# Fusion kernel on one core: Gate's weights multiplied into the second layer's weights, and the logits taken as 8 more columns of the second layer from the second block on

## What is computed

```python
h = x @ w_in
g = np.where(h > 0.0, h, alpha * (np.exp(np.minimum(h, 0.0)) - 1.0))
x2 = g @ w_out                       # 1536 x 384
logits = x2 @ w_gate                 # 1536 x 8
expert_idx = np.argmax(logits, axis=1)
probs = np.exp(logits - logits.max(-1, keepdims=True))
probs /= probs.sum(-1, keepdims=True) + 1e-09
gate_w = probs[np.arange(N), expert_idx]
# a token's row goes to the next free slot of its expert (capacity 384); then per expert
# out = gate_w * (max(row @ w1, 0) @ w2)
```

## Time and profile before

| | us |
|---|---|
| runs of the kernel before (3) | 440.31, 440.59, 441.05; median 440.59 |
| the profiled execution: time | 441.02 |
| the profiled execution: span of the trace | 439.3 |
| PE busy in it | 418.8 (95%) |
| VectorE, ScalarE, GpSimd busy | 244.7, 183.2, 232.5 |
| mean granted clock of PE | 0.999 |

### The profile page before, as it was taken

The page is one execution under the profiler, slowest core; times in us unless marked ns, Lnnn a source line. Parts: engine busy times, 40 slices in busy tenths (PEclk is TensorE's granted clock), DMA queues, the critical chain, the costliest instruction groups (busy, mean ns, idle before and its releaser), DMA issues.

```text
span 439.3 us, 9249 instructions
## 1 busy us (share of the span) xinstructions
PE 418.8 (95%) x3604; PEld 399.6 (91%) x3604; DVE 244.7 (56%) x595; ACT 183.2 (42%) x390; POOL 232.5 (53%) x240
## 2 busy tenths in 40 slices
PE   7779999999999999999999999988999999999994
PEld 7669989999999999899999999866999999999994
DVE  7867864665466536744664477573455365463521
ACT  4356643333332333233333445334455564564520
POOL 1888776549554965396533334114343825627431
PEclk9999999999999999999999999999999999999999
DMA  6993978204210411030008000721826638458100
GB/s 242 399 411 87 367 247 297 76 17 131 64 49 17 133 52 60 1 101 2 1 15 327 1 1 37 286 91 31 313 95 265 244 127 328 152 196 313 44 30 26
DMA packets 16825, 62.36 MB, mean 142 GB/s; under 512 B 2044, under 2 KB 9510, under 8 KB 14737
## 3 DMA queue, kind: packets, MB, share of 16 engines
q1 hardware_dynamic: 14992, 57.08, 36.1%
q0 software_dynamic: 1792, 4.73, 2.9%
HBM read 49.38 MB, written 13.21 MB: 142 GB/s over the span
## 4 chain that ended last, share of the span: by engine, by line
PE 65%; DVE 11%; POOL 9%; issue 8%; ACT 3%; DMA 3%; SPq 0%; POOLq 0%; DVEq 0%; ACTq 0%
PE bank L1193 18%; PE bank L1195 18%; PE bank L1194 17%; POOL g_lo L596 3%; ACT elu L726 2%; DVE elu L1027 2%; PE bank L1355 2%; DVE wd_lo L922 2%; DMA rkt<-rkt 1%; POOL slots L574 1%; DVE wd_lo L928 1%; DMA nat<-nat 1%; DVE elu L1030 1%; PE bank L1342 1%; POOL rku L518 1%
## 5 line engine op out<-in xcount | busy, mean ns | idle before, releaser
L596 POOL TENSOR_TENSOR g_lo<-elu,g_hi 128x256 fp32r<-128x256 f32 x95 | 75.1, 790 | 99.5 <-ACT g_hi L728 98.3
L726 ACT ACTIVATE elu<-elu 128x256 f32<-128x256 f32 x96 | 40.2, 419 | 109.3 <-DVE elu L1027 109.0
L1193 PE MATMUL bank<-xt,wd_hi 128*128 128x256 f32 x288 | 81.7, 284 | 4.0 <-DVE elu L1030 2.0
L1195 PE MATMUL bank<-xt,wd_lo 128*128 128x256 f32 x288 | 81.0, 281 | 0.0
L1194 PE MATMUL bank<-xt,wd_hi 128*128 128x256 f32 x288 | 81.0, 281 | 0.0
L1193 PE MATMUL bank<-wd_hi,g_hi 128*128 128x384 f32 x192 | 67.4, 351 | 0.0
L1030 DVE SCALAR_TENSOR_TENSOR elu<-elu,bank 128x256 f32<-128x256 f32 x96 | 40.4, 421 | 47.9 <-ACT elu L726 47.9
L1027 DVE TENSOR_SCALAR elu<-bank 128x256 f32<-128x256 f32 x96 | 40.3, 420 | 47.0 <-PE bank L1195 46.6
L1194 PE MATMUL bank<-wd_lo,g_hi 128*128 128x384 f32 x192 | 64.5, 336 | 0.0
L1195 PE MATMUL bank<-wd_hi,g_lo 128*128 128x384 f32 x192 | 64.4, 336 | 0.0
L1193 PEld LDWEIGHTS bank<-xt,wd_hi 128*128 128x128 f32 x288 | 54.1, 188 | 6.2 <-DVE elu L1030 3.3
(11 more groups left out here) (199 smaller groups left out, 956.6 us busy)
## 6 DMA issues: line engine op xcount, KB each, us to landing
we_raw<-wexp SPq DMA_DIRECT2D x8, 1536.0 KB, 7.1
wd_raw<-wexp SPq DMA_DIRECT2D x8, 1536.0 KB, 7.5
nat<-nat SPq DMA_DIRECT2D x10, 672.0 KB, 4.9
rkt<-rkt SPq DMA_DIRECT2D x12, 512.0 KB, 6.8
xrow<-slots SPq DMA_DIRECT2D x16, 193.0 KB, 7.3
wd_raw<-win SPq DMA_DIRECT2D x4, 768.0 KB, 8.6
wd_raw<-wout SPq DMA_DIRECT2D x4, 768.0 KB, 10.6
slots<-blank SPq DMA_DIRECT2D x1, 2702.0 KB, 12.6
```

The lines of the kernel that those rows point to most:

```text
L596: nc.gpsimd.tensor_tensor(g_lo[:, f % 4, :], elu[:, f % 2, :], g_hi[:, f % 4, :].bitcast(F32), ALU.subtract).then_inc(s_glo, 1)
L726: nc.scalar.activation(elu[:, f % 2, :], elu[:, f % 2, :], ACT.Exp).then_inc(s_exp, 1)
L1193: mm(dst, w_hi, x_hi, start=start, stop=False)
L1195: return mm(dst, w_lo, x_hi, start=False, stop=stop)
```

## The change

Gate's weights are multiplied into w_out on the chip, once, in block 0: for this SP loads the transposed w_out (3.1 MB, `wo_tr`), and PE runs 12 plain f32 products of 32 by 512 (`gated_w_out`, tile 11), ScalarE copies the result, PE transposes it in four pieces (`gated_transpose`, tile 13), and ScalarE and VectorE split it into 8 columns that stand ahead of the 384 of each tile of w_out in `wd_hi` and `wd_lo` (128 x 16 x 8 numbers). The rows of w_out in these tables are thus 392 long (`WO`), and the four loads of w_out land in pieces of 384 numbers. Gate's weights are padded to 32 columns. From block 1 on `fc2` has 392 columns, and the logits are the first 8 columns of the copied rows (`x2row`, now 394 long). Only the logits of block 0, in block 1, are still made by transposes and products of their own. For the later blocks the transposes, their copies and the logits' products are gone, and the routing steps move: `shift` to tile 3, `choose` 5, `gates` 6, `count` 7, `place_rows` 8, the scatters 9 and 10. After block 5 the same steps are gone, the others keep their order. The diff, cut to its core:

```diff
+    WO = NE + DM
+    GP = 32
+    NG = 128 // GP
+    GCOL = DFF // NG
...
-    gate_w = new("gate_w", [128, KT, NE])
+    gate_w = new("gate_w", [128, KT, GP])
-    x2row = [new(f"x2row{b}", [128, BT, XR]) for b in range(2)]
+    x2row = [new(f"x2row{b}", [128, BT, NE + XR]) for b in range(2)]
...
-    wd_hi = new("wd_hi", [128, 2 * WI], F32R)
+    wd_hi = new("wd_hi", [128, WI + FT * WO], F32R)
...
-        F_T, F_LG, F_CHOOSE, F_GATE, F_CNT, F_SLOT, F_SCAT = 3, 6, 7, 8, 8, 9, 10
+        F_T, F_LG = 3, 6
+        F_WG, F_WGT = 11, 13
+        def route(n):
+            return dict(zip(("shift", "choose", "gates", "count", "place", "scatter"),
+                            (6, 7, 8, 8, 9, 10) if n == 0 else (3, 5, 6, 7, 8, 9)))
...
             def load_out(i):
                 cols = slice(i * WCOL, (i + 1) * WCOL)
-                sp.dma_start(wd_raw[:, WI + i * WCOL:WI + (i + 1) * WCOL], wout[:, cols]).then_inc(s_wld2[i], 16)
+                at = WI + i * WCH * WO
+                sp.dma_start(wd_raw[:, at:at + WCH * WO].rearrange("p (f c) -> p f c", f=WCH)[:, :, NE:WO],
+                             wout[:, cols].rearrange("p (f c) -> p f c", f=WCH)).then_inc(s_wld2[i], 16)
...
             for c in range(4, NSTEP):
                 load_rkt(c)
+                if c == 4:
+                    sp.dma_start(wo_tr[:, :, :], wouttr).then_inc(s_wtl, 16)
                 load_nat(c)
...
+            def gated_copy():
+                act.wait_ge(s_wg, 1)
+                nc.scalar.copy(wg_tr[:, :], ps_s[0][:, :]).then_inc(s_wgt, 1)
+            def gated_hi():
+                act.wait_ge(s_wgb, 1)
+                nc.scalar.copy(gate_part(wd_hi), gate_bank()).then_inc(s_wghi, 1)
...
+            def gated_lo():
+                dve.wait_ge(s_wghi, 1)
+                V.tensor_tensor(gate_part(wd_lo), gate_bank(), gate_part(wd_hi).bitcast(F32),
+                                ALU.subtract).then_inc(s_wglo, 1)
...
-                dve.wait_ge(s_lg, n + 1)
-                L = ps_lg.rearrange("p (t e) -> p t e", t=BT)
+                if n == 0:
+                    dve.wait_ge(s_lg, 1)
+                    L = ps_lg.rearrange("p (t e) -> p t e", t=BT)
+                else:
+                    for t in range(BT):
+                        dve.wait_ge(s_x2[t], n + 1)
+                    L = x2row[n % 2][:, :, 0:NE]
...
-                cols = w_out_cols(f)
+                cols = gated_cols(f) if n else w_out_cols(f)
                 for t in range(BT):
                     g = slice(t * C, (t + 1) * C)
-                    last = product(ps_x2[t][:, 0:DM], g_hi[:, f % 4, g], g_lo[:, f % 4, g], wd_hi[:, cols],
+                    last = product(ps_x2[t][:, x2_cols(n)], g_hi[:, f % 4, g], g_lo[:, f % 4, g], wd_hi[:, cols],
                                    wd_lo[:, cols], f == 0, f == FT - 1)
...
+            def gated_w_out():
+                pe.wait_ge(s_gw, 16)
+                pe.wait_ge(s_wtl, 16)
+                pe.wait_ge(s_att, 8)
                 for kt in range(KT):
-                    last = nc.tensor.transpose(ps_s[t][:, 128 * kt:128 * kt + 128], x2row[n % 2][:, t, 128 * kt:128 * kt + 128],
+                    for g in range(NG):
+                        last = mm(ps_s[0][GP * g:GP * (g + 1), :], gate_w[:, kt, :], wo_tr[:, kt, GCOL * g:GCOL * (g + 1)],
+                                  start=kt == 0, stop=kt == KT - 1, skip_group_check=True)
+                last.then_inc(s_wg, 1)
...
-            for t in range(BT):
-                x2_transpose(NB - 1, t)
             tile_fc1(0, 0, 2, s_ah, 1)
-            logits(NB - 1)
             tile_fc1(0, 1, 0, s_ah, 1)
```

More of the change, by code:

```diff
@@ L59, in build @@
     assert FE == 2 * HALF == ET * C == 4 * SN and SN == 2 * C and 0 < EB < NB - 1
+    assert NE <= GP and GCOL == 4 * 128 and FT == 4 * NG and WO <= 512
     assert N1 * ECH == W1 and H <= 8 and BT * NE <= 64
@@ L210, in build @@
         s_blank = sem("blanks_written")
+        s_wtl = sem("w_out_turned_loaded")
+        s_wg = sem("gated_w_out_done")
+        s_wgt = sem("gated_w_out_copied")
+        s_wgb = sem("gated_w_out_transposed")
+        s_wghi = sem("gated_w_out_hi_ready")
+        s_wglo = sem("gated_w_out_lo_ready")
         s_h = sem("h_done")
@@ L352, in w_out_cols, with gated_cols, x2_cols, w_out_pair @@
         def w_out_cols(f):
-            return slice(WI + f * DM, WI + (f + 1) * DM)
+            return slice(WI + f * WO + NE, WI + (f + 1) * WO)
+        def gated_cols(f):
+            return slice(WI + f * WO, WI + (f + 1) * WO)
+        def x2_cols(n):
+            return slice(NE if n == 0 else 0, WO)
+        def w_out_pair(t, i):
+            return t[:, WI + i * OCH * WO:WI + (i + 1) * OCH * WO].rearrange("p (f c) -> p f c", f=OCH)[:, :, NE:WO]
+        def gate_part(t):
+            return t[:, WI:WI + FT * WO].rearrange("p (g i c) -> p i g c", g=NG, c=WO)[:, :, :, 0:NE]
+        def gate_bank():
+            return ps_s[1][:, :].rearrange("p (i g e) -> p i g e", g=NG, e=GP)[:, :, :, 0:NE]
         def half_of(a, b):
@@ L734, in _ @@
                         x2_rows(n - 1)
-                    if n and f == F_T + 1:
-                        x2_transposed(n - 1)
-                    if n and f == F_CHOOSE:
+                    if n == 1 and f == F_T + 1:
+                        x2_transposed()
+                    if n and f == route(n - 1)["choose"]:
                         probs(n - 1)
@@ L741, in _ @@
                         x_hi(c)
+                    if n == 0 and f == F_WG + 1:
+                        gated_copy()
+                    if n == 0 and f == F_WGT + 1:
+                        gated_hi()
                     if n == NB - 1 and f >= F_E0 - 1 and (f - F_E0) % 2:
@@ L1052, in _ @@
                         x2_rows(n - 1)
-                    if n and f == F_T + 1:
-                        x2_transposed(n - 1)
-                    if n and f == F_LG:
+                    if n == 1 and f == F_T + 1:
+                        x2_transposed()
+                    if n and f == route(n - 1)["shift"]:
                         shift(n - 1)
-                    if n and f == F_CHOOSE:
+                    if n and f == route(n - 1)["choose"]:
                         choose(n - 1)
-                    if n and f == F_GATE:
+                    if n and f == route(n - 1)["gates"]:
                         gates(n - 1)
-                    if n and f == F_SLOT:
+                    if n and f == route(n - 1)["place"]:
                         place_rows(n - 1)
+                    if n == 0 and f == F_WGT + 1:
+                        gated_lo()
                     if n == NB - 1 and f >= F_E0:
@@ L1355, in logits @@
                         last = mm(ps_lg[:, NE * t:NE * (t + 1)], x2t[:, t, 128 * kt:128 * kt + 128],
-                                  gate_w[:, kt, :], start=kt == 0, stop=kt == KT - 1)
+                                  gate_w[:, kt, 0:NE], start=kt == 0, stop=kt == KT - 1)
                 last.then_inc(s_lg, 1)
@@ L1379, in _ @@
                         back(c)
-                    if n and f == F_T:
+                    if n == 0 and f == F_WG:
+                        gated_w_out()
+                    if n == 0 and f == F_WGT:
+                        gated_transpose()
+                    if n == 1 and f == F_T:
                         for t in range(BT):
-                            x2_transpose(n - 1, t)
-                    if n and f == F_LG:
-                        logits(n - 1)
-                    if n and f == F_CNT:
+                            x2_transpose(t)
+                    if n == 1 and f == F_LG:
+                        logits()
+                    if n and f == route(n - 1)["count"]:
                         count(n - 1)
```

78 lines of the change are left out of this document (46 added, 32 removed).

## The result

The changed kernel takes 433.93 us (median of 4 runs, 433.57 to 435.54); the kernel before, run beside it on the same chip, 440.82 (4 runs, 440.31 to 442.23). The ratio is 0.9846, with an interval from 0.9812 to 0.988. The profiled execution took 434.17 us with a span of 432.5, against 441.02 and 439.3 before: 6.8 us less. Forecast were 433.3 us and 7.3 us less.

A forecast was written before the change was run, and what follows sets the result against it. TensorE (PE) was taken to bound the kernel, busy 418.8 of 439.3 us. Terms: -9.55 + 1.65 + 3.0 + 0.2 - 2.6 = -7.3 us, so the median 440.59 becomes 433.3, range 431.5 to 434.6 (chance 0.64).

The forecast's parts named there:

- Transposes and logits, 0.63 and 1.33 a block: Blocks 2 to 5: removing six transposes saves 0.63 us and the logits 1.33 each; 2.5 and 5.3 us for four.
- The columns, 3.4 ns each product: Blocks 1 to 5: 480 second-layer products of 392 instead of 384 columns add 3.4 ns each, 1.65 us.
- Waits of block 5, 0.8: Block 5: moved routing steps remove PE's 0.58 wait for one-hot rows and half of 0.43 for an activation: 0.8 us.
- rival 1: Block 5: VectorE takes PE's place, logits' 1.3 and the 0.8 not gained: 435.4 us; chance 0.13, shared with a half-packed product.
- more than 1 us: Block 5, sign that the forecast is wrong: VectorE as PE's releaser for more than 1 us in all.
- Block 0, 3.0: Block 0 grows: 2.6 us for the delay handed on through VectorE to z, plus 0.4 for four transposes.
- four at a time (strips by turns): Block 0's product of weights: four strips of 32 rows by turns, like the attention's, so 10.3 / 4 = 2.6 us.
- Transfers, 0.2: Block 0: the 3.1 MB are hidden in the idle queue; w_out's smaller pieces ahead of nat of chunk 2 cost 0.2 us.
- The end, 2.6: After the last block: the count, held by PE's four product groups, and the steps behind it come 2.6 us earlier.
- 2 (10.3 us for the product): Block 0: the product does not run four at a time, 7.7 us more, 441.0, no measurable change; chance 0.04.
- 3 (a step for the width or pitch): Second layer's 480 products pay a step for new width or pitch; from 19 ns each nothing is gained; chance 0.05.
- 4 (transfers hold nat): Block 0: the 3.1 MB hold nat of chunk 3 until 42, GpSimd waits some 6 us, 439.3; chance 0.05 with partial forms.

The follow-up runs named there:

- the last runs: Changed kernel with the weights' product in PE's wait for z: 433.7 us; then also two filling products instead of six: 431.73; then one: 430.78.

## Why the prediction came out as it did

The time measured, 433.93 us, lies 0.6 above the forecast of 433.3 and inside its own range of 431.5 to 434.6; by the spans the sum of 7.3 us was 0.5 too large. Point by point:

- **Transposes and logits, 0.63 and 1.33 a block**: right. With the old waits and the wider products, blocks 2 and 3 were to shrink by 1.98 and 2.23 us and shrank by 2.05 and 2.29. "An instruction taken off PE is time off the kernel" held there.
- **The columns, 3.4 ns each product**: right in the mean distance. In block 1, where they stand alone, the block grew by 0.07 us and not 0.33. Its first three tiles still run the second layer of block 0, so it has 78 wide products and not 96, which is 0.27. Against these stand a wait for the row numbers that went (0.08 at 95.33 in before) and a step that got shorter by 0.11 (at 106.72), for a reason that isn't shown.
- **Waits of block 5, 0.8**: the step that failed. Old waits of 1.15 us went (the two of 0.58 and 0.43, and the 0.14 for ScalarE's copy), but three new ones of 0.82 came, so 0.33 was gained. These 0.47 are most of the miss in blocks 4 and 5, which gave 3.3 us instead of 4.1; the other 0.25 wasn't traced. I had asked what is late next on VectorE (rival 1) and got its part about right (0.51 us of activation waits, below the "more than 1 us" that would have spoken for it). I had not asked what PE would wait for at the place of the removed transposes: the copy that they too had waited for, 0.31 us now against 0.14.
- **Block 0, 3.0**: close, in part by luck. Wait for the mask 0.40 (0.35), product 2.71 (2.6), transposes 0.42 (0.4), and 0.37 given back; they add to 3.16 of the 3.27 measured. The forecast contradicts itself here: it hands PE's delay of 2.95 on to VectorE in full and then counts 2.6. Counted in full, block 0 would have been 3.35. What gave back 0.37 was a split of VectorE that took 0.95 instead of 1.32 us, which no part of the forecast had. Nor was VectorE's step at 53.10 waiting for PE: its own split had ended just then, 0.04 us after PE's product. The product run twice confirms that PE's delay is handed on. By the Trainium skill, "TensorE: Matmul & The Clock Gate", Measured speedup vs the span model, it would have been 3.2 us; measured are 24 x 0.43 / 2.71 = 3.8 at a time, so the share of the ideal that its figure for three tiles gives (0.79) was too low for these four. The reason that I gave for four at a time (strips by turns) was right only by half: without turns it is not one at a time.
- **Transfers, 0.2**: the cost was right (0.1 to 0.2), the path to it was not. I took the issue times of before; with four times the pieces of w_out ahead of them, nat and gate_w took 5.5 us to issue where they had taken 0.9. The idle stretch of the queue had room for it, and the 3.1 MB landed 2.5 us later than forecast, with 6 us to spare.
- **The end, 2.6**: 2.75. The count was bound by PE's four groups as worked out and came 2.68 us earlier; the steps from there to h's second half took 0.08 less.
- **Rivals**: 2 (10.3 us for the product), 3 (a step for the width or pitch) and 4 (transfers hold nat) did not come; 3 is excluded by the runs with the new pitch and with 400 columns, 1 came in a small part. Rival 4 met a weaker test than it was written for: the 3.1 MB were issued only at 28.1, and nat of chunk 3 landed at 34.3.

The change leaves two gains lying, which the last runs take up: PE's wait for z in block 0, and filling products that cover a chain now shorter. Together they give 430.78 us, 2.4% below before (ratio 0.9757) where the change as made gives 1.5%.

## What to carry to other kernels

- When an instruction is taken off the engine that binds, ask what the instruction behind it then waits for. Here it was a copy that ran beside them, and 0.17 us of the 0.63 that the transposes were worth in block 5 did not come.
- A one-off preparation, such as the product of weights here, costs its full length where the next engine is waiting for the same one, however many waits that engine has later; put it into the wait itself, and its followers early enough that they don't hold the next bank.
- Fillers are sized to a stretch. When the stretch in front of them shrinks, they are the next thing to cut: from the first filler to the experts it was 4.98 us with six and 1.94 with one. Look at the granted clock with each cut: with one it stayed at 1.00 in this stretch.

## What the runs showed of the hardware

- **Strips of 32 output rows behave like four queues.** In one strip, f32 records of 512 columns follow at 0.43 us; different strips overlap almost fully. Six orders of the same product (2.71, 3.59, 5.29, 5.33, 13.87 and 15.63 us) fit one count: handed out in order, four records (or two products) held by each strip. It is a model that fits, two of the six foretold; that each strip holds four is read from times only. For the programmer: of these orders turns between strips were the fastest, and by the count a strip that is given more than four records in a row holds up the others.
- Weight loads of different strips overlap running products. The timeline of after's product has them in fours (x4), one four for each step of 0.43 us:

```profile
51.66 0.15 PEld L1411 LDWEIGHTS bank<-wo_tr,gate_w 128*32 128x32 f32 x4 [0.27 <-issue]
52.08 0.16 PEld L1411 LDWEIGHTS bank<-wo_tr,gate_w 128*32 128x32 f32 x4 [0.27 <-issue]
```

  The Trainium skill, "TensorE: Matmul & The Clock Gate", What overlaps and what doesn't, says that this happens only where the row group differs. Here all records use all 128 rows, so the measurement differs from it, and it decides. It isn't special to strips either: over the whole span PEld is busy for 91% and PE for 96%, and most products use all rows.
- **Many small pieces hold up the issuing of what follows.** w_out in pieces of 1536 bytes left nat and gate_w 2.0 to 3.5 us to issue (before 0.37 and 0.56), in the changed kernel and in the old kernel with the new pitch alike. In the latter gate_w is still the 12 KB of the earlier trace rows, so it isn't gate_w's size. The bytes of w_out are the same in all three; the pieces are four times as many.
- **The clock can dip in one trace and not in the next.** The same wait of 1.47 us of PE was followed by 3.4 us at 0.5 of the clock in the run with two fillers (products of 384 columns 0.32 us apart), and by none in after and in the runs with six and with one. A comparison of single traces should look at the granted clock of each first.
